# Retention attention on one core: TensorE's work of a unit grouped into two tile shapes

## What is computed

```python
def _attn_ref(q, k, v):                      # q, k, v: (4, 8, 768, 64)
    gamma = 1.0 - 2.0 ** (-5.0 - np.arange(H))
    scale = 1.0 / np.sqrt(D)
    for t in range(S):
        state = gamma[None, :, None, None] * state + np.einsum('bhd,bhe->bhde', k[:, :, t], v[:, :, t])
        y[:, :, t] = scale * np.einsum('bhd,bhde->bhe', q[:, :, t], state)

def _moe_ref(x, modality_id, w_gate, modality_bias, w1, w2):   # x: (3072, 512), 8 experts
    logits = x @ w_gate + modality_bias[modality_id]
    e_idx = np.argmax(logits, axis=1)
    ...                                      # softmax weight gate_w of the chosen expert
    out[mask] = gate_w[mask, None] * (np.maximum(x[mask] @ w1[e], 0.0) @ w2[e])

def _moe2_ref(x, w1, w2, w3, w_out):
    return (((x @ w1) * (x @ w2)) @ w3) @ w_out
```

## Time and profile before

| | |
|---|---|
| median of 3 runs | 900.5 us (900.22 to 901.03) |
| the profiled execution: its time | 901.14 us |
| its span, first to last instruction | 899.4 us |
| mean granted TensorE clock | 0.989 of full |
| busy shares of the span | PE 96%, PEld 82%, DVE 32%, ACT 27%, POOL 10% |
| chain of work that ended last | PE 93%, DVE 3%, issue 2%, ACT 1% |

### The profile page before, as it was taken

The page is one execution under the profiler, slowest core; times in us unless marked ns, Lnnn a source line. Parts: engine busy times, 40 slices in busy tenths (PEclk is TensorE's granted clock), DMA queues, the critical chain, the costliest instruction groups (busy, mean ns, idle before and its releaser), DMA issues.

```text
span 899.4 us, 13770 instructions
## 1 busy us (share of the span) xinstructions
PE 867.2 (96%) x5356; PEld 733.9 (82%) x5357; DVE 286.9 (32%) x495; ACT 243.4 (27%) x412; POOL 86.1 (10%) x107
## 2 busy tenths in 40 slices
PE   7999999998979999999998999999999999999995
PEld 5777778787979998888888788888888888888884
DVE  3656678630212234121327331121221230230210
ACT  2334423321212243211326322222221221231210
POOL 2222002202020120202000001001001001001001
PEclk9999999998989999999999999999999999999998
DMA  9999861323030343202045102002002002001000
GB/s 332 392 343 297 292 233 47 141 95 96 1 95 0 93 159 121 71 22 65 28 152 175 47 1 82 12 1 83 12 0 87 6 0 94 0 0 47 1 13 35
DMA packets 43481, 84.76 MB, mean 94 GB/s; under 512 B 7728, under 2 KB 7728, under 8 KB 43440
## 3 DMA queue, kind: packets, MB, share of 16 engines
q1 hardware_dynamic: 33376, 60.33, 19.3%
q0 software_dynamic: 4736, 14.72, 5.1%
q10 hardware_dynamic: 5328, 9.13, 2.9%
HBM read 63.16 MB, written 21.00 MB: 94 GB/s over the span
## 4 chain that ended last, share of the span: by engine, by line
PE 93%; DVE 3%; issue 2%; ACT 1%; DMA 0%; ACTq 0%; POOL 0%; DVEq 0%
PE bank L388 46%; PE attn L388 33%; PE bank L747 3%; PE attn L784 3%; PE pair L756 2%; PE pair L854 1%; PE bank L796 1%; PE attn L775 1%; PE pair L762 1%; PE pair L768 1%; PE bank L906 1%; DMA qkv<-in_q_t_dram 0%; DVE we_p L974 0%; DVE w3T L974 0%; ACT we_p L560 0%
## 5 line engine op out<-in xcount | busy, mean ns | idle before, releaser
L388 PE MATMUL bank<-yT,wab 128*128 128x512 f32 x1152 | 262.2, 389 | 1.7 <-issue 1.7
L388 PEld LDWEIGHTS bank<-yT,wab 128*128 128x128 f32 x1152 | 216.2, 188 | 46.6 <-issue 1.9
L388 PE MATMUL bank<-xT,we_p 128*128 128x512 f32 (+2 forms) x768 | 155.6, 364 | 12.2 <-issue 8.4
L388 PEld LDWEIGHTS bank<-xT,we_p 128*128 128x128 f32 x768 | 138.2, 194 | 29.2 <-issue 10.9
L388 PE MATMUL attn<-hT,we_p 128*128 128x512 f32 (+2 forms) x768 | 153.5, 357 | 0.0
L388 PEld LDWEIGHTS attn<-hT,we_p 128*128 128x128 f32 x768 | 132.9, 188 | 14.4
L388 PE MATMUL attn<-wc,gT 128*128 128x512 f32 x576 | 131.5, 389 | 0.0
L388 PEld LDWEIGHTS attn<-wc,gT 128*128 128x128 f32 x576 | 108.2, 188 | 22.4
L1255 DVE TENSOR_TENSOR g<-bank,acopy 128x512 f32<-128x512 f32 x48 | 33.2, 691 | 258.9 <-PE bank L388 258.9
L1216 DVE SCALAR_TENSOR_TENSOR hT<-bank,hT 128x512 fp32r<-128x512 f32 x64 | 44.1, 690 | 173.5 <-ACT hT L635 173.5
L635 ACT ACTIVATE hT<-bank 128x512 fp32r<-128x512 f32 x64 | 38.2, 598 | 116.0 <-PE bank L388 116.0
(11 more groups left out here) (154 smaller groups left out, 560.7 us busy)
## 6 DMA issues: line engine op xcount, KB each, us to landing
we_raw<-in_moe_w_dram SPq DMA_DIRECT2D x6, 2048.0 KB, 8.9
yT_sorted<-yout ACTq DMA_DIRECT2D x8, 1024.0 KB, 4.9
qkv<-in_q_t_dram SPq DMA_DIRECT2D x24, 256.0 KB, 3.8
qkv<-in_v_dram SPq DMA_DIRECT2D x24, 256.0 KB, 5.4
x_rows<-x_keep SPq DMA_DIRECT2D x24, 256.0 KB, 5.5
ytile<-yT_sorted SPq DMA_DIRECT2D x6, 1024.0 KB, 5.0
qkv<-in_k_t_dram SPq DMA_DIRECT2D x23, 256.0 KB, 5.3
qkv<-in_k_dram SPq DMA_DIRECT2D x20, 256.0 KB, 6.0
```

The costliest lines, as they stand in the source:

```text
L388: i = pe.matmul(out_, left(a), right(b), start=(first and n == 0), stop=(last and n == 2), **kw)
```

## The change

`scores` computes in eight tiles of 64x64 a pair of heads at a time where it had 64x128: the 128 keys are cut in two halves (index a), 16 matmuls for 8. It runs a unit ahead: the scores of unit u+1 stand at the head of unit u, those of unit 0 ahead of the loop. `prob` has two buffers for that. `from_state` follows it directly. `rows`, `gates` and `logit_rows` are gone; `rows_and_logits` does their work in 8 matmuls of 128x64: the stationary operand is half of the tokens of `xTu`, the moving one `iw`, the identity with the 8 gate columns beside it (136 columns). The partial logits thus come out with tokens on partitions, and neither ACT's copy to `lTu` nor the second transpose is there. `from_chunk` and `update` (now of the same unit) follow. On the DVE `masked` comes first in a unit, `keep_logits` and `new_state` are those of unit u-2, and `qdecay` is that of the unit itself. ACT's `keep` waits for `keep_logits` (`s_lg`). POOL fills the identity part of `iw` with four copies at the start. SP's list is as it was.

```diff
--- before.py
+++ after.py
@@ -50,7 +50,8 @@
     NX = NI + GT + 1
     LAG = B + 1
     RANKED = 4
-    SQ = 32
+    HALF = P // 2
+    XW = P + E
     XCH = 16
     NW = (NI + 3 * E) // GT
     MINW = NT // GT
@@ -114,7 +115,7 @@
         small = fixed("small", [P, small_w])
         sm = {n: small[:, a:a + w] for n, (a, w) in small_at.items()}
         ident = sm["ident"]
-        w_gate_t = fixed("w_gate_t", [P, KD, SQ])
+        iw = fixed("iw", [P, KD, XW])
         logits = fixed("logits", [P, E, NT])
         meta_in = fixed("meta_in", [P, NT, 2])
         row_id = fixed("row_id", [P, NT], I32)
@@ -142,12 +143,11 @@
         r = region(at_r)
         state = r("state", [P, B, HP, D])
         qdk = r("qdk", [P, 2, HP, P])
-        prob = r("prob", [P, 2, HP, P])
+        prob = r("prob", [P, 2, 2, HP, P])
         kdk = r("kdk", [P, 2, H, D])
         maskt = r("maskt", [P, 2, HP, P])
         qdect = r("qdect", [P, HP, P])
         xTu = r("xTu", [P, KD, P])
-        lTu = r("lTu", [P, P])
 
         x_keep = region(at_i)("x_keep", [P, NT, DM])
         at_s = at_i + NT * DM * 4
@@ -239,9 +239,8 @@
         s_xTu = sem("s_xTu")
         s_up = sem("s_up")
         s_state = sem("s_state")
+        s_ident = sem("s_ident")
         s_xl = sem("s_xl")
-        s_gt = sem("s_gt")
-        s_lt = sem("s_lt")
         s_lg = sem("s_lg")
         s_keep = sem("s_keep")
 
@@ -494,8 +493,9 @@
         @block.gpsimd
         def _(pool):
             pool.memset(zero[:, :], 0.0).then_inc(s_zero, 1)
-            pool.memset(w_gate_t[:, :, :], 0.0).then_inc(s_zero, 1)
             pool.wait_ge(s_const, 16)
+            for j in range(KD):
+                pool.tensor_copy(iw[:, j, 0:P], ident).then_inc(s_ident, 1)
             kdec = sm["kdec"].rearrange("p (c h) -> p c h", c=C)
 
             def kdecay(c, b, u):
@@ -555,16 +555,14 @@
         def _(act):
             act.dma_start(qkv[:, 0, KT, :], slot_v[KT][0, 0, :, :]).then_inc(s_ldq[0], 16)
             act.dma_start(small[:, :], c_small).then_inc(s_const, 16)
-            act.wait_ge(s_zero, 2)
-            act.dma_start(w_gate_t[:, :, 0:E], w_gate.rearrange("(c p) e -> p c e", p=P)).then_inc(s_gatew, 16)
+            act.wait_ge(s_zero, 1)
+            act.dma_start(iw[:, :, P:XW], w_gate.rearrange("(c p) e -> p c e", p=P)).then_inc(s_gatew, 16)
             copy = lambda o, i, **kw: act.activation(o, i, ACT.Copy, **kw)
 
             def keep(u):
 
-                act.wait_ge(s_xl, u + 1)
-                copy(lTu[:, :], pair[:, 0:1, P:2 * P].rearrange("p a t -> p (a t)")).then_inc(s_gt, 1)
-                dst = x_keep[:, u, :]
-                copy(dst.rearrange("p (j t) -> p j t", j=KD), pair[:, :, 0:P]).then_inc(s_keep, 1)
+                act.wait_ge(s_lg, u + 1)
+                copy(x_keep[:, u, :].rearrange("p (j t) -> p j t", j=KD), pair[:, :, 0:P]).then_inc(s_keep, 1)
 
             def w3_hi(f, halves=range(2)):
                 for j in halves:
@@ -737,37 +735,35 @@
             def out_rows(j, r):
                 return head_rows(r ^ (j % 2))
 
-            def scores(c, b, u, start):
+            def halves(a):
+                return slice(a * HALF, (a + 1) * HALF)
+
+            def scores(c, b, u):
                 pe.wait_ge(s_ldq[b], 32 * (c + 1))
-                if not start:
+                if u:
                     pe.wait_ge(s_prob, u)
                 for j in range(HP):
-                    t = slice(j * P, (j + 1) * P)
-                    for r in range(2):
-                        i = pe.matmul(bank[2 + r][:, t], qkv[head_rows(r), b, KT, t], qkv[head_rows(r), b, QT, t], start=True, stop=True)
+                    for a in range(2):
+                        keys = slice(j * P + a * HALF, j * P + (a + 1) * HALF)
+                        for r in range(2):
+                            i = pe.matmul(bank[2 + r][halves(a), j * P:(j + 1) * P], qkv[head_rows(r), b, KT, keys],
+                                          qkv[head_rows(r), b, QT, j * P:(j + 1) * P], start=True, stop=True, skip_group_check=True)
                 i.then_inc(s_qk, 1)
 
-            def rows(u):
+            def rows_and_logits(u):
                 pe.wait_ge(s_xTu, u + 1)
                 if u:
                     pe.wait_ge(s_keep, u)
-                    pe.wait_ge(s_lg, u)
+                else:
+                    pe.wait_ge(s_gatew, 16)
+                    pe.wait_ge(s_ident, KD)
                 for j in range(KD):
-                    pe.transpose(pair[:, j, 0:P], xTu[:, j, :], ident)
-
-            def gates(u):
-                if u == 0:
-                    pe.wait_ge(s_gatew, 16)
-                for j in range(KD):
-                    i = pe.matmul(pair[j * SQ:(j + 1) * SQ, 0, P:2 * P], w_gate_t[:, j, :], xTu[:, j, :], start=True, stop=True, skip_group_check=True)
+                    for a in range(2):
+                        i = pe.matmul(pair[halves(a), j, 0:XW], xTu[:, j, halves(a)], iw[:, j, :], start=True, stop=True, skip_group_check=True)
                 i.then_inc(s_xl, 1)
 
-            def logit_rows(u):
-                pe.wait_ge(s_gt, u + 1)
-                pe.wait_ge(s_keep, u + 1)
-                pe.transpose(pair[:, 2, P:2 * P], lTu[:, :], ident).then_inc(s_lt, 1)
-
             def from_state(b, u):
+                pe.wait_ge(s_xTu, u)
                 pe.wait_ge(s_qdk, u - B + 1)
                 pe.wait_ge(s_state, u - B + 1)
                 for j in range(HP):
@@ -781,7 +777,7 @@
                 for j in range(HP):
                     for r in range(2):
                         h = 2 * j + r
-                        i = pe.matmul(attn[out_rows(j, r), r, j // 2 * P:(j // 2 + 1) * P], qkv[:, b, V, h * D:(h + 1) * D], prob[:, r, j, :],
+                        i = pe.matmul(attn[out_rows(j, r), r, j // 2 * P:(j // 2 + 1) * P], qkv[:, b, V, h * D:(h + 1) * D], prob[:, u % 2, r, j, :],
                                       start=(first and j < 2), stop=(j >= HP - 2), skip_group_check=True)
                 i.then_inc(s_yTu, 1)
 
@@ -798,20 +794,17 @@
                 i.then_inc(s_up, 1)
 
             def unit(c, b, u):
-                scores(c, b, u, u == 0)
-                if 0 < u <= NT - B:
-                    update((b - 1) % B, u - 1, u <= B)
-                if u == 1:
-                    pe.wait_ge(s_const, 16)
-                if u:
-                    rows(u - 1)
-                    gates(u - 1)
+                if u + 1 < NT:
+                    scores(c + (b + 1) // B, (b + 1) % B, u + 1)
                 if c:
                     from_state(b, u)
+                if u:
+                    rows_and_logits(u - 1)
                 from_chunk(c, b, u, c == 0)
-                if u:
-                    logit_rows(u - 1)
-
+                if c < C - 1:
+                    update(b, u, c == 0)
+
+            scores(0, 0, 0)
             each_unit(unit)
 
 
@@ -838,12 +831,7 @@
                 pe.matmul(bank[6][:, 0:E * NT], sm["before"], chosen, start=True, stop=True)
                 pe.matmul(bank[7][:, 0:E * NT], sm["ones"], chosen, start=True, stop=True).then_inc(s_cnt, 1)
 
-            def last_rows():
-                rows(NT - 1)
-                gates(NT - 1)
-
-            w3_product(0, {1: last_rows, 4: lambda: logit_rows(NT - 1)})
-
+            w3_product(0, {2: lambda: rows_and_logits(NT - 1)})
 
             def x_rows(w, chunks):
                 pe.wait_ge(s_xin, w * (16 * GT) + 16 * GT)
@@ -989,15 +977,14 @@
             def masked(u):
 
                 dve.wait_ge(s_qk, u + 1)
-                tt(prob[:, 0, :, :], bank[2][:, :].rearrange("p (j t) -> p j t", j=HP), maskt[:, 0, :, :], ALU.mult)
-                tt(prob[:, 1, :, :], bank[3][:, :].rearrange("p (j t) -> p j t", j=HP), maskt[:, 1, :, :], ALU.mult).then_inc(s_prob, 1)
+                for r in range(2):
+                    i = tt(prob[:, u % 2, r, :, :], bank[2 + r][:, :].rearrange("p (j t) -> p j t", j=HP), maskt[:, r, :, :], ALU.mult)
+                i.then_inc(s_prob, 1)
 
             def keep_logits(u):
 
-                dve.wait_ge(s_lt, u + 1)
-                at = (logits[:, :, u:u + 1] if isinstance(u, int) else logits[:, :, bass.ds(u, 1)]).rearrange("p e n -> p (e n)")
-                parts = pair[:, 2:3, P:2 * P].rearrange("p a (j e) -> p (a e) j", j=KD)
-                dve.tensor_reduce(at, parts[:, 0:E, :], AX.X, ALU.add).then_inc(s_lg, 1)
+                dve.wait_ge(s_xl, u + 1)
+                dve.tensor_reduce(logits[:, :, u:u + 1].rearrange("p e n -> p (e n)"), pair[:, :, P:XW].rearrange("p j e -> p e j"), AX.X, ALU.add).then_inc(s_lg, 1)
 
             def qdecay(c, b):
                 dve.wait_ge(s_ldq[b], 32 * (c + 1))
@@ -1013,17 +1000,17 @@
 
             def unit(c, b, u):
 
+                masked(u)
                 if u > 1:
                     keep_logits(u - 2)
-                masked(u)
-                if 0 < u <= NT - B:
-                    if u == 1:
```

(10 more changed lines are left out.)

## The result

The changed kernel takes 897.0 us in the median of 10 runs (891.6 to 900.6) against 900.2 of the kernel before in the same sessions; the ratio is 0.996, with a 95% interval of 0.994 to 0.998. It is faster, by 3.3 us where 12 were forecast, and its runs scatter over 9 us where those of before scatter over 3 (almost 6 in a later set of 17). The clock seems to have a part in that: the two shortest runs, 891.6 and 894.3 us, have a mean granted clock of 0.994 of full, the other eight 0.990 to 0.993, and a difference of 0.003 is 2.7 us of 897 by my estimate. The profiled execution took 897.1 us (span 895.4), 4.0 less than the profiled one of before.

The account below looks back on a forecast made before the run. TensorE's own list was taken to bound the first stage; 901.1 - 10.7 (stage) - 1.2 (behind it) = 889.2 us, with the median 0.6 lower at 888.6. The forecast's own range was 886 to 892, 8 in 10 884.5 to 896.

Parts of the forecast that it names:

- What bounds the kernel before: First stage: TensorE's own list sets its length from unit 1 on; PE busy in 96% of the span.
- The gap belongs to the change of shape: Between TensorE's matmul groups: about 0.15 us comes with a change of tile shape, not with every new group.
- The start: First stage, ahead of unit 1: unit 1 starts at 15.1 us, bounds 14.3 to 16.2.
- The end of the stage: First L388, behind unit 23: starts at 101.2 us against 111.9 before, -10.7.
- 16 x 3.92: Stage sum's term for middle units 4 to 19: 3.92 us each, where 4.53 was.
- Unit 23: Last unit of the first stage, without next scores: 2.57 us.
- DVE and ACT: Beside TensorE in the first stage: costed at nothing; their ring in units 20 to 22 0 to 0.5 us in all.
- Behind the stage: Last logits and counts after the first stage: earlier sums pass on -1.2 us, bounds 0.3 and 1.6.
- Transfers: First-stage loads keep up, 3.90 us a unit at 403 GB/s; rival that they become the bound: +7, 896, chance 0.11.
- the third: Rival: TensorE can't be handed its MATMULs so fast; 0.059 us each, some 925 us, chance 0.05.
- L796 to L775: Kernel before, 44 MATMULs from 96.84 to 99.00 us: 0.049 each, taken against the rival of slow instruction supply.
- The clock: Rival: the half-clock stretch behind a pause in the expert windows changes, -2.5 to +2 us; chance 0.06.

Follow-up runs that it names:

- e10: Kernel before with q, k, v loads cut to 32 of 128 partitions from chunk 1 on; only first stage compared: unit 4.53 us, stage end 111.99 against 111.90.
- e4: Changed kernel with q, k, v loads cut to 32 of 128 partitions (64 KB) from chunk 1 on; only first stage compared, ending at 103.28 us.
- e11: Second run of the e4 kernel (changed kernel, 64 KB q, k, v loads from chunk 1 on); first stage ends at 102.98 us.
- e5: e1 with the chunk product of unit 0 set ahead of the scores of unit 1; 892.9 us, ratio 0.9907 to the kernel before.
- e1: Changed kernel with scores again 8 matmuls in 64x128 tiles, still a unit ahead; 894.2 us, ratio 0.9926 to the kernel before.
- e3: Changed kernel with scores in 64x128 and x rows with logits in 128x128; 895.6 us, ratio 0.9948 to the kernel before.

## Why the prediction was wrong, point by point

- **What bounds the kernel before**: right. e10 took half of the bytes away and moved nothing.
- **The gap belongs to the change of shape**: right. With two changes a unit takes 3.89 us (3.92 forecast), with three 4.10 and 4.08, with four 4.30. The third and fourth cost 0.2 each, a little over the 0.15 to 0.16 taken.
- **The start**: right. Unit 1 at 14.84 for 15.1.
- **The end of the stage**: wrong, 110.1 for 101.2, and the step that failed is the sum itself, "16 x 3.92", which has every unit at its streaming time and lets only waits on engines and data stand against it. The late arrival of TensorE's own instructions is put at nothing there; units 4 to 19 took 7.6 us more than the 62.7 of the sum. Units 5, 6, 10, 11 and 18 took 5.36, 5.15, 6.10, 5.22 and 5.63 us: 8.0 more than 5 x 3.89. A pause costs more than its idle time: 1.04 idle in unit 5 cost 1.47, since the idle is counted from the end of the matmuls in flight. With the same instructions and light loads (e4, e11) each of these units takes 3.89.
- **Unit 23**: mis-sized. Without next scores at its head the state product waits for `xTu` of unit 22, 0.7 to 1.0 us in every variant of the changed kernel. I had `xTu` under the cover of scores everywhere; in this unit there are none. Units 22 and 23 together took 7.49 us for 6.02, with 0.3 us of a pause in it.
- **DVE and ACT**: put at nothing (0 to 0.5 us), and in the changed kernel's own profile no wait for them shows outside unit 23. But the account of the DVE left out the bias computation in unit 7; where no pause gives it time, in e4 and e11, it costs TensorE 0.75 us of waiting, and unit 8 takes 4.87.
- **Behind the stage**: right. -1.0 at the counts, -1.4 at the first expert window (-3.2 in all less the stage's 1.8), for -1.2.
- **Transfers**: the queue kept up, as forecast (0.4 us of waits for k), and this was the wrong question. I weighed 1.57 MB a unit against the loads' own lead, and not what else travels over the same engines.
- **The rivals**: the third, that TensorE can't be handed the instructions so fast, had the right object and the wrong mechanism. I priced it as a steady rate, 0.059 us a MATMUL and +25 us, gave it 0.05, and took L796 to L775 as evidence against it. That evidence holds: e4 and e11 run the whole list at 0.0405 us a MATMUL. But a short stretch says nothing on supply by pieces, where the loss comes at most once a piece and with weight only beside full queues. The Trainium skill has the mechanism (Runtime: NRT & Kernel Launch, Instruction fetch mechanics: blocks of 16 KiB, 256 instructions, fetched by a DMA queue of the engine's own) and says that the fetch stays hidden because dispatch is slower than it. The trace agrees with the first (16 KB packets on q8, and pauses 248 to 250 LDWEIGHTS and MATMULs apart) and not with the second: 6.6, 5.6 and 6.7 us of pauses.
- **The clock**: the stretch at half clock in the expert windows did come out shorter, part of the 2 us gained between 166 and 293 us; that was within the range. The range itself failed by 1 us at its upper end, since it took this loss from no row.

## What to carry to other kernels

Count instructions next to time when matmuls are made smaller: float32 matmuls in 64x64 tiles double the LDWEIGHTS and MATMULs for the same streaming, and TensorE's list travels over the DMA engines as well. A gap of 0.15 us at a change of shape is cheaper than 32 more instructions in a stage that keeps those engines full. And where a sum puts a group at its streaming time, look in the DMA view of the trace for the instruction queue, how far apart its packets are and how fast the new list uses one up.

## What the runs showed of the hardware

- TensorE pauses in the middle of a group for 0.2 to 2.0 us, marked issue, behind a late 16 KB packet on the instruction queue, and goes on 1.2 to 1.8 us after the packet's end. It happened at 42 or more LDWEIGHTS and MATMULs a us in every profile with a DMA share of 0.92 or more, at 39 a us in e5 and not in e1, and at 33 or 34 a us not in the kernel before or e3, and once, for 0.2 us, in e10.
- The packet took 0.9 to 1.6 us at light and at full traffic alike. Its start, counted from the place where the piece before is used up, came 3.1 to 3.4 us later in the median at a DMA share of 0.96 to 1.01, and 0.7 to 1.1 at 0.55 to 0.58.
- 32 float32 MATMULs of 128 columns in 64x64 tiles, four at a time, take 0.93 us to the next start; 16 in 64x128 tiles, two at a time, take 1.09 with the change of shape behind them (e1).
- A change of tile shape costs 0.13 to 0.21 us, and a new group of the same shape with waits of its own at most 0.05 (0.93 and 0.97 us for the scores and the x rows, where the streaming is 0.88 and 0.94).
